# Reordering the exponential, the ELU operation and the first transposes in an attention and two-MLP kernel

## The reference

```
x = attn(x, softmax(weight_gen))            # 7 taps, 8 heads
h = x @ moe_w_in;   g = max(0.01*h, h);                     x = g @ moe_w_out
h = x @ moe2_w_in;  g = where(h>0, h, exp(min(h,0)) - 1);   x = g @ moe2_w_out
```

## Time and profile before

| | before |
|---|---|
| median of 3 runs | 1184.88 us (1182.89 to 1187.18) |
| the profiled execution, its own time | 1186.27 us |
| its span on the core | 1183.6 us |
| granted TensorE clock, mean | 0.998 |
| busy PE / ACT / DVE / POOL | 1160.1 / 750.1 / 661.4 / 422.3 us |

### The profile page before, as it was taken

How to read it: one execution, slowest core, us unless ns; L and a number is a source line. 1 busy time by engine, 2 the same in 40 slices (tenths; PEclk the granted TensorE clock), 3 DMA queues, 4 the chain that set the end, 5 groups by cost and what they waited for, 6 DMA issues and landing times.

```text
span 1183.6 us, 22757 instructions
## 1 busy us (share of the span) xinstructions
PE 1160.1 (98%) x9808; PEld 927.1 (78%) x9808; DVE 661.4 (56%) x690; ACT 750.1 (63%) x846; POOL 422.3 (36%) x409
## 2 busy tenths in 40 slices
PE   6899999999999999999999999999999999999998
PEld 4777887878878777887878878778787878878776
DVE  6766736456474554636446374564736556364554
ACT  3566757567575665657666575665757657575665
POOL 5727531707135090541806226080440806200000
PEclk9999999999999999999999999999999999999999
DMA  5312021020101101021020110201121020110000
GB/s 171 115 50 67 25 78 28 28 79 22 57 28 47 59 28 52 28 78 28 28 66 27 65 28 28 79 28 52 28 78 28 28 65 22 34 28 28 15 28 27
DMA packets 44724, 55.45 MB, mean 47 GB/s; under 512 B 4117, under 2 KB 32915, under 8 KB 44625
## 3 DMA queue, kind: packets, MB, share of 16 engines
q1 hardware_dynamic: 44624, 54.01, 14.8%
HBM read 36.29 MB, written 17.69 MB: 46 GB/s over the span
## 4 chain that ended last, share of the span: by engine, by line
PE 87%; DVE 4%; ACT 3%; POOL 3%; issue 2%; DMA 1%; SPq 0%; POOLq 0%
PE y_a_rows L617 27%; PE hidden L549 27%; PE y_b L610 19%; PE hidden L553 9%; PE hidden L578 5%; DVE hid_lo L1125 2%; DVE act L1100 2%; ACT hid_hi L915 1%; ACT act L899 1%; POOL mix L325 1%; POOL prod L313 1%; DMA wk<-in_weight_gen_dram 0%; ACT ya L873 0%; DMA xw<-in_x_dram 0%; POOL prod L337 0%
## 5 line engine op out<-in xcount | busy, mean ns | idle before, releaser
L617 PE MATMUL y_a_rows<-hid_hi,dn 64*128 64x512 f32 x2048 | 574.7, 392 | 0.0
L610 PE MATMUL y_b<-hid_hi,dn 64*128 64x512 f32 x1024 | 401.5, 392 | 0.5 <-PE y_b L610 0.2
L610 PE MATMUL y_b<-hid_lo,dn 64*128 64x512 f32 x1024 | 400.9, 392 | 0.0
L617 PEld LDWEIGHTS y_a_rows<-hid_hi,dn 64*128 64x128 f32 x2048 | 332.5, 185 | 44.8
L617 PE MATMUL y_a_rows<-hid_lo,dn 64*128 64x512 f32 x1024 | 359.2, 391 | 0.0
L1125 DVE TENSOR_TENSOR hid_lo<-hidden,hid_hi 128x1024 fp32r<-128x1024 f32 x128 | 156.5, 1222 | 231.4 <-ACT hid_hi L915 231.2
L1125 DVE TENSOR_TENSOR hid_lo<-act,hid_hi 128x1024 fp32r<-128x1024 f32 x127 | 169.8, 1337 | 178.4 <-ACT hid_hi L915 176.7
L897 ACT ACTIVATE hidden<-hidden 128x1024 f32<-128x1024 f32 x127 | 128.2, 1009 | 184.5 <-PE hidden L553 184.5
L313 POOL TENSOR_TENSOR mix<-xw,wk 128x384 f32<-128x384 f32 x30 | 39.0, 1301 | 571.8 <-DVE wk L1041 566.3
L899 ACT ACTIVATE act<-hidden 128x1024 f32<-128x1024 f32 x127 | 130.3, 1026 | 141.7 <-PE hidden L553 135.3
L549 PE MATMUL hidden<-in_a_hi,up_a_hi 64*128 64x512 f32 x1020 | 205.5, 399 | 7.2 <-DVE act L1100 3.4
(11 more groups left out here) (104 smaller groups left out, 1189.4 us busy)
## 6 DMA issues: line engine op xcount, KB each, us to landing
xw<-in_x_dram SPq DMA_DIRECT2D x14, 960.0 KB
raw_b<-squares_out SPq DMA_DIRECT2D x60, 96.0 KB, 2.2
out_dram<-staged SPq DMA_DIRECT2D x15, 384.0 KB, 2.5
squares_in<-prod SPq DMA_DIRECT2D x56, 96.0 KB, 2.0
squares_out<-ya SPq DMA_DIRECT2D x15, 256.0 KB, 2.0
raw_a<-squares_in SPq DMA_DIRECT2D x14, 256.0 KB, 2.8
raw_d<-in_moe_w_out_dram SPq DMA_DIRECT2D x8, 384.0 KB, 3.4
raw_a<-in_moe_w_in_dram SPq DMA_DIRECT2D x8, 256.0 KB, 3.7
```

The lines of the kernel that those rows point to most:

```text
L610: return nc.tensor.matmul(y_b[:, :], dn[m][rows, f, P:2 * P], v[rows, s % HB, HALF[i]], start=start, stop=stop)
L617: return nc.tensor.matmul(bank[:, :], dn[m][rows, f, first:first + P], v[rows, s % HB, HALF[i]], start=(f == 0 and n == 0), stop=(f == FT ...
```

## The change

Four edits.

1. **ELU steps.** ACT's order in step s becomes relu(s), exp(s), rounding(s-1), and DVE's becomes elu(s), rests(s-1). The waits stay.
2. **Mixing of chunk 0.** The fourth term gets a place of its own in unused columns of `act` (`term4`, `term5`), product 6 goes to `staged_rows`, and the two waits for PE's reading of the first two terms (`s_termu`) go.
3. **Softmax of chunk 1.** `softmax_a(1)` moves behind the mixing share of chunk 0, two splits of weights and `mlp1_input_lo(0, 0)` on DVE, `softmax_exp(1)` behind `mlp1_input_hi(0, 1)` on ACT. Two warming matmuls (`WARM`, L789) go.
4. **Transposes of chunk 1.** Their first part moves from the end of step 6 to the end of step 7 of phase 0, the second from the end of step 7 to behind `down` of step 5 at the head of phase 1. `down` of steps 6 and 7 is redistributed: step 6 now stands ahead of `up` of g = 8, step 7 lies inside step s = 1, and step s = 2 of phase 1 has `up` alone. On ACT and DVE `mlp1_input_hi/lo(1, 0)` moves behind the rounding and the rests of step 7.

```diff
-        FIRST_TERMS = ((prod, 1), (prod2, 2), (mix, 5), (prod, 10))
+        FIRST_TERMS = ((prod, 1), (prod2, 2), (mix, 5), (term4, 10))
...
-            eng.wait_ge(s_termu, 1)
-            product(4, prod)
+            product(4, term4)
+            product(5, term5)
             eng.wait_ge(done, 5)
-            product(5, staged_rows)
-            eng.wait_ge(s_termu, 2)
-            product(6, prod2)
+            product(6, staged_rows)
...
@@ PE, phase
-                    if known(ph) and ph == 1 and s == 0:
-                        pe.wait_ge(s_lo, g - LAG + 1)
-                        down_open(of, step, g - LAG)
-                        down_close(of, step, g - LAG)
+                    if ph == 1 and s == 0:
+                        pe.wait_ge(s_lo, g - 2)
+                        down_open(0, ST - 3, g - 3)
+                        down_close(0, ST - 3, g - 3)
+                        transpose_mix(1, 1)
+                        pe.wait_ge(*down_split(0, DN_PARTS - 1))
+                        pe.wait_ge(s_lo, g - 1)
+                        down_open(0, ST - 2, g - 2)
+                        down_close(0, ST - 2, g - 2)
...
-                    if known(ph) and (ph == 0 and s < LAG or ph == 1 and s == 0):
+                    if ph == 0 and s < LAG or ph == 1 and s in (0, 2):
+                        up(m, input_of(m, c), g, s, True)
+                        continue
+                    if ph == 1 and s == 1:
+                        pe.wait_ge(s_lo, g - 1)
+                        down_open(0, ST - 1, g - 2)
+                        down_close(0, ST - 1, g - 2)
                         up(m, input_of(m, c), g, s, True)
                         continue
...
-                    if s in (6, 7) and known(ph) and ph == 0:
-                        transpose_mix(1, s - 6)
+                    if ph == 0 and s == 7:
+                        transpose_mix(1, 0)
-            for _ in range(WARM):
-                nc.tensor.matmul(y_a[0][:, 0:P], ident[:, :], ident[:, :], start=True, stop=True)
@@ ACT, phase
                     else:
+                        exponential(c, s)
                         if s:
                             rounding(1, c, g - 1, s - 1)
-                        exponential(c, s)
+                    if (ph, s) == (0, 7):
+                        mlp1_input_hi(1, 0)
@@ ACT, ahead of the phases
             softmax_exp(0)
-            softmax_exp(1)
             round_up(0, 0)
             round_up(0, 1)
             mlp1_input_hi(0, 0)
             mlp1_input_hi(0, 1)
+            softmax_exp(1)
@@ DVE, phase
                     else:
+                        activation(c, s)
                         if s:
                             rests(1, g - 1, s - 1)
-                        activation(c, s)
+                    if (ph, s) == (0, 7):
+                        mlp1_input_lo(1, 0)
@@ DVE, ahead of the phases
-            softmax_a(1)
             mixing_share()
             split_up(0, 0)
             split_up(0, 1, (0,))
             mlp1_input_lo(0, 0)
+            softmax_a(1)
             mlp1_input_lo(0, 1)
             softmax_b(1)
```

More of the change, by code:

```diff
@@ L96, in attention_leaky_elu_mlps @@
         xw = sb("xw", [P, PAD + J, D], f32)
-        wk = [sb(f"wk{n}", [P, J * H, TAPS], f32) for n in (0, 1)]
+        wk = [sb("wk0", [P, J * H, TAPS], f32)]
         wmax = sb("wmax", [P, J * H], f32)
@@ L124, in attention_leaky_elu_mlps @@
         staged = sb("staged", [P, 2, 2 * D], f32)
+        wk.append(sb("wk1", [P, J * H, TAPS], f32))
         staged_rows = staged[:, :, :].rearrange("p a (j d) -> p (a j) d", j=J // 2)
+        spare = act[:, :, :].rearrange("p a n -> p (a n)")[:, T:T + 2 * J * D].rearrange("p (a j d) -> p a j d", a=2, j=J)
+        term4, term5 = spare[:, 0], spare[:, 1]
         hidden = ps("hidden", [P, 2, 2 * T])
@@ L154, in attention_leaky_elu_mlps @@
         s_termv = sem("first_mix_steps_vector")
-        s_termu = sem("first_mix_terms_summed")
         s_turna = sem("first_mix_128_features")
@@ L220, in attention_leaky_elu_mlps @@
         EARLY = 2
-        WARM = 2
         J_POOL = 1
@@ L348, in first_mixing @@
             add(mix, staged_rows)
-            eng.wait_ge(s_termu, 1)
-            product(4, prod)
+            product(4, term4)
+            product(5, term5)
             eng.wait_ge(done, 5)
-            product(5, staged_rows)
-            eng.wait_ge(s_termu, 2)
-            product(6, prod2)
+            product(6, staged_rows)
             eng.wait_ge(done, 7)
-            add(prod, staged_rows)
+            add(term4, term5)
             eng.wait_ge(done, 9)
-            add(prod, prod2)
+            add(term4, staged_rows)
         def split_down(eng, ops, m, n):
@@ L706, in sum_first_mix @@
                         last = nc.tensor.matmul(by_token(turn_b)[:, j], term[:, j, P:D], ident[:, :], start=False, stop=(end and j == J - 1))
-                    last.then_inc(s_mixt if end else s_termu, 1)
+                    if end:
+                        last.then_inc(s_mixt, 1)
             def transpose_mix(c, part):
@@ L768, in phase @@
                         pe.wait_ge(*down_split(1, DN_PARTS - 1))
-                    if known(ph) and ph == 1 and s == 1:
-                        pe.wait_ge(*down_split(0, DN_PARTS - 1))
                     pe.wait_ge(s_lo, g - LAG + 1)
@@ L950, in phase @@
                         continue
-                    if known(ph) and (ph, s) in ((0, 7), (1, 0)):
-                        mlp1_input_hi(1, ph)
+                    if (ph, s) == (1, 0):
+                        mlp1_input_hi(1, 1)
                     if s == LAG - 1 and dm is not None:
@@ L1135, in phase @@
                         continue
-                    if known(ph) and (ph, s) in ((0, 7), (1, 0)):
-                        mlp1_input_lo(1, ph)
+                    if (ph, s) == (1, 0):
+                        mlp1_input_lo(1, 1)
                     if s == LAG - 1 and dm is not None:
```

## The result

The kernel after takes 1203.88 us (median of 4 runs, 1202.19 to 1204.87), the one before 1185.24 us in the same session: a ratio of 1.0157 [1.0135, 1.0179]. A second timing in another session gave 1202.82 us and 1.0104 [1.0089, 1.0119]; the kernel before took 1190.61 us in that one. The kernel before moves more from run to run (1183 to 1192 us over all sessions) than most others do, so differences between variants are taken from the variants' own medians where that is possible.

A forecast was written before the change was run, and what follows sets the result against it. PE, busy 98% of the span, was taken to bound the kernel. From 1186.3 us: -7.0 for the start, +36 for edit 1, +12 for the clock gave 1227, 1225 for the median; range 1200 to 1240.

The forecast's parts named there:

- the start: Chunk 0 and 1 mixing, softmax and transposes: stalls and low clock go, one wait comes; -7.0 us, bounds -4 and -9.
- edit 1: ELU phases: late handovers and last phase +36 us, clock falls +12 us.
- the new wait: Step 2 of phase 1 has `up` alone; the next `up` waits for the rests of g = 9: 1.5 us lost.
- the ring: ELU steps: relu, exp, elu, rests and the next relu wait in a circle, 4.60 us a turn where PE needs 4.42.
- The handover: From ELU to next LReLU phase: DVE's input comes late, PE 2.6 us later at 13, 1.4 at one.
- the two bounds: PE's start of the next phase: 1.4 us later without POOL beside DVE, 2.6 us later with it.
- The picture of taking turns: At the phase change DVE and POOL alternate operations, stretching rests and L1052; PE 2.6 us later, not 1.4.
- The clock: After PE's stalls of about 3.1 us between phases the clock falls 7 times at 1.7 us: +12 us.
- the half: Clock falls taken after 7 of the 14 phase changes, between bounds of none (0) and all (24 us).
- the rival that nearly all fall: The clock falls after nearly all phase changes: 1237 us, chance 0.16.
- (a) to (d): Clock never falls: 1213, 0.22; handover 1 us late: 1192-1195, 0.10; handover not late: 1170, 0.06; start gives nothing: 1230, 0.06.

The follow-up runs named there:

- experiment 1: The kernel before with only the allocation of tile `wk1` moved behind `staged`: 1165.03 us, ratio 0.9804.
- (4): The kernel after with the ELU step order put back to the old one; the other edits and the moved `wk1` stay: 1157.62 us, ratio 0.9741.
- Experiment 5: The kernel after with a third `act` buffer from chunk 1 on, so relu(s) waits for rests(s-3); chunk 0 keeps the old order: 1158.05 us, ratio 0.9742.
- experiment 3: The kernel before with only the new ELU step order, on the old layout: 1239.88 us, ratio 1.0436.
- experiment 6: The kernel after with `softmax_b` of chunk c + 3, and so POOL's mixing, at s = 7 instead of s = 5: 1185.58 us, ratio 0.9981.
- (a): The kernel before with 128 unused bytes per partition ahead of `in_a_hi0`: 1164.72 us, ratio 0.9800.
- (c): The kernel before with 384 unused bytes per partition ahead of `in_a_hi0`: 1164.28 us, ratio 0.9778.

## Why the prediction was right in sign and wrong in size

**The step that failed is the one that isn't in the sum.** The prediction took "a free step is 4.42 us" from the earlier trace rows and held it fixed. In the kernel after it is 4.307, worth 1188.16 - 1165.03 = 23.1 us (experiment 1). The terms as measured, from one variant to the next: from 1188.2 -23.1 for the layout (experiment 1), -7.4 for the start (4), +46.3 for edit 1 (the kernel after). That this ends at 1203.9 is so by construction and proves nothing; what it gives is the size of each term. Forecast were 0, -7.0 and +48. With the first term added the forecast would have been 1202, within 2 us of the time. Some of that closeness is luck: on the layout that the prediction had in mind edit 1 costs 51.7 us and not 48, because the clock fell at all 14 handovers. The missing term is no mere size: nothing in the trace of before has a row for it. But the diff had the line, and a price of nothing for it was never argued.

**Edits 2 to 4.** Right in sum: -7.4 for -7.0, both waits gone, the clock at the start kept. Two parts were off and nearly cancel: `up` gets its `in_b` at 22.34 for 23.99, 1.7 us earlier and not 2.2, and the new wait is 1.03 for 1.5.

**Edit 1, the ring.** Right: 81 waits for "70 to 80", turns of 4.60 for 4.60. Experiment 5 shows it by taking it away: the ring gone, 46 us come back. That `up` doesn't feel the ring ahead of the handover holds on the old layout (steps 4 to 6 take 4.41 to 4.42 us in experiment 3) and not on the new one: in the kernel after, steps 5 and 6 of the phase shown take 4.43 and 4.60 us for 4.31. PE's wait for elu at step 4 is gone; one of 1.0 us is left, near the end.

**The handover.** Forecast 2.6 us for each period, of which the two bounds gave 1.4 to the ring and 1.2 to POOL. Measured 2.2 on the old layout (experiment 3) and 2.5 on the new one (72.39 - 69.90), where PE arrives earlier and the ring doesn't. POOL's share is 0.8 (experiment 6), so on the new layout the ring had 1.7, more than forecast, and POOL less; on the old one the two weren't taken apart. The picture of taking turns fits the rows: rests and L1059 are stretched and elu isn't (1.22 us at 343.61, beside POOL's 0.86), and L1059, begun at 346.21, ends 0.55 us behind the end of POOL's two operations at 344.24 + 2.66 = 346.90, where it takes 0.68 without POOL. The Trainium skill (GPSIMD Engine Reference, section 1, Specifications) names DVE's instructions in a 2-port mode or with two SBUF inputs as the ones that contend with POOL. Rests and L1059 have two SBUF inputs, and elu has one of its inputs in PSUM; these rows agree.

**The clock.** Forecast 7 falls at 1.7 us; there were 5 at 1.6 with the new layout and 14 at 1.7 with the old one. Both the half and the rival that nearly all fall were open, and which came depended on a change outside edit 1. The gaps hardly differ in length (2.8 to 2.9 us and once 2.15 where all fell, 2.8 to 3.0 and once 2.2 where 5 did), so the length of the gap alone doesn't decide it. By the Trainium skill (TensorE: Matmul & The Clock Gate, Part 1), the low rate is the default that activity releases; experiment 3 fits what the prediction made of that, a fall at each handover, and the kernel after does not. What picks the 5 is not settled.

**The rivals.** (a) to (d) all kept the step at 4.42, and none of them held. That the time came out near the lower end of the range is due to a gain that no case had; without it the same edits would come to about 1232 us (1188.2 - 7.4 + 51.7, an estimate from experiments 3 and 4), in the upper part of the range.

## What to carry to other kernels

Read the allocation lines of a diff like its instructions: a tile added or removed moves everything behind it, and here the operands' place was worth 23 us of 1188, three times what the start edits gave. Where two experiments differ in layout, first compare the time of a stretch in which the engine never waits. Bringing an operation forward in an in-order queue puts something else back: follow the buffer that the later one frees, count the links of the ring that this closes (4.60 us against a step of 4.31), and if the ring is the slower, add a buffer with the reordering or leave it. Then look at what the moved work runs beside: the third buffer alone only won back the loss, and the gain of 12.9 us came when POOL's mixing was moved as well.

## What the hardware showed that was not expected

PE's rate with two 64-row matmuls at a time depended on where in SBUF the streamed tiles start. A pair takes 4.307 / 19 = 226.7 ns at remainders of 256 and 512 bytes modulo 1024, and 4.418 / 19 = 232.5 ns at 128. The Trainium skill (TensorE: Matmul & The Clock Gate, Part 1) gives about 215.7 ns from start to start for 512 columns at the full clock, for single matmuls back to back and not for such pairs; both are above it. Only these three remainders were tried, the stationary tiles weren't moved, and whether 1024 is the right modulus or the step goes with some smaller one is not told apart: all that is shown is that with all the streamed tiles at 128 PE is slow, at 256 and 512 fast, and with the inputs at 128 and `hid_*` at 256 between. `act` moved along with them in experiment 1 and in (a) and (c), but PE doesn't read it, and ACT's and DVE's work beside PE made no difference to the pairs. The mechanism stays open.

DVE's busy time rose with the faster layout at the same 690 instructions, from 661.4 us to 675.6 in experiment 1. The two traces say where: 13.5 of these 14 us are in three groups, `in_b<-yb,in_b` (11.6 to 17.8 us), `in_a_lo<-ya,in_a_hi` (13.4 to 18.0) and `hid_lo<-act,hid_hi` (171.2 to 173.9). All three read two tiles in SBUF, and in each more of its time lies beside a busy POOL than before, 2.9 to 9.3 us in the first. So it is most likely the same contention as at the handover, met more often because the timing moved; no run tests it, and it is off the path there.
